# Hidden rows of an expert layer turned by way of DRAM and VectorE, with the second layer two slots behind

## The reference, cut to what matters

```python
e_idx = np.argmax(x @ w_gate, axis=1)              # x: 1536 x 512
for e in range(8):
    mask = e_idx == e
    h = np.maximum(x[mask] @ w1[e], 0.0)           # w1[e]: 512 x 1024
    ye = h @ w2[e]                                 # w2[e]: 1024 x 512
    out[mask] = gate_w[mask, None] * eom[mask, e, None] * ye
```

## Time and profile before

| | |
|---|---|
| median of 3 runs | 767.78 us (767.4 to 767.9) |
| span of the profiled execution | 765.7 us |
| TensorE busy | 754.3 us, 99% |
| VectorE, ScalarE, GpSimd busy | 421.5, 345.6, 368.7 us |
| expert stage (TensorE, first `layer1` to last `layer2`) | about 253 to 494 us |

### The profile page before, as it was taken

How to read it: one execution, slowest core, us unless ns; L and a number is a source line. 1 busy time by engine, 2 the same in 40 slices (tenths; PEclk the granted TensorE clock), 3 DMA queues, 4 the chain that set the end, 5 groups by cost and what they waited for, 6 DMA issues and landing times.

```text
span 765.7 us, 12544 instructions
## 1 busy us (share of the span) xinstructions
PE 754.3 (99%) x4243; PEld 630.2 (82%) x4243; DVE 421.5 (55%) x842; ACT 345.6 (45%) x658; POOL 368.7 (48%) x253
## 2 busy tenths in 40 slices
PE   8999999999999999999999999999999999999996
PEld 7677777777776788888888888998899889989985
DVE  8777777777765645444444545588147126414710
ACT  7766677777764313442244210285047117404610
POOL 5866567878721899777887860244200120010001
PEclk9999999999999999999999999999999999999998
DMA  4534333222111867755675611520200010000000
GB/s 112 128 97 121 92 81 100 57 59 57 28 45 27 324 205 255 219 182 184 213 246 157 233 54 32 194 92 1 61 22 1 29 56 1 0 28 15 1 14 28
DMA packets 42781, 73.70 MB, mean 96 GB/s; under 512 B 20352, under 2 KB 24096, under 8 KB 42720
## 3 DMA queue, kind: packets, MB, share of 16 engines
q1 hardware_dynamic: 29632, 30.05, 13.4%
q10 hardware_dynamic: 9584, 31.53, 12.4%
q0 software_dynamic: 3504, 11.30, 4.6%
HBM read 60.48 MB, written 11.28 MB: 94 GB/s over the span
## 4 chain that ended last, share of the span: by engine, by line
PE 62%; issue 29%; POOL 2%; DVE 2%; ACT 2%; DMA 1%; SPq 0%; POOLq 0%; DVEq 0%
PE pair_s L1478 14%; PE pair_t L1493 14%; PE pair_u L1284 8%; PE bank_b L1299 8%; PE pair_s L1271 5%; PE pair_t L1271 4%; PE pair_u L1453 2%; PE bank_b L1324 1%; POOL out L646 1%; PE pair_s L1531 1%; DVE g_lo L1213 1%; PE bank_a L1240 1%; POOL y_raw L640 1%; POOL w_part L518 1%; PE bank_a L1444 1%
## 5 line engine op out<-in xcount | busy, mean ns | idle before, releaser
L518 POOL TENSOR_TENSOR w_part<-w_raw,w_part 128x1024 fp32r<-128x1024 f32 x80 | 190.2, 2408 | 57.5 <-ACT w_part L756 57.3
L756 ACT ACTIVATE w_part<-w_raw 128x1024 fp32r<-128x1024 f32 x72 | 73.9, 1054 | 126.4 <-PE pair_t L1493 101.4
L1580 PE MATMUL pair_t<-w_part,g_hi 128*128 128x512 f32 x384 | 119.0, 391 | 0.3 <-POOL w_part L518 0.3
L646 POOL DMA_INDIRECT out<-o_sb,token x12 | 11.8, 985 | 208.5 <-DVE o_sb L1183 208.5
L1493 PE MATMUL pair_t<-w_part,hid_t 128*128 x456 | 109.0, 394 | 0.0
L1478 PE MATMUL pair_s<-w_part,xs_t 128*128 x456 | 108.7, 394 | 0.2 <-issue 0.2
L1478 PEld LDWEIGHTS pair_s<-w_part,xs_t 128*128 128x128 f32 x456 | 84.3, 188 | 17.7 <-issue 0.9
L1493 PEld LDWEIGHTS pair_t<-w_part,hid_t 128*128 128x128 f32 x456 | 84.4, 189 | 16.8
L859 ACT ACTIVATE elu<-elu 128x384 f32<-128x384 f32 x64 | 33.6, 525 | 122.9 <-DVE elu L1203 122.8
L698 ACT ACTIVATE exps<-exps,nmax 128x768 f32<-128x768 f32 x96 | 88.5, 925 | 0.6 <-DVE exps L916 0.6
L1580 PEld LDWEIGHTS pair_t<-w_part,g_hi 128*128 128x128 f32 x384 | 71.6, 188 | 15.1 <-issue 0.7
(11 more groups left out here) (219 smaller groups left out, 1088.3 us busy)
## 6 DMA issues: line engine op xcount, KB each, us to landing
w_raw<-in_moe_w ACTq DMA_DIRECT2D x48, 512.0 KB, 6.2
w_raw<-in_moe_w SPq DMA_DIRECT2D x16, 512.0 KB, 5.6
ys_sorted<-ys SPq DMA_DIRECT2D x19, 256.5 KB, 3.6
w_raw<-in_moe_w_in ACTq DMA_DIRECT2D x8, 512.0 KB, 5.7
raw<-in_q SPq DMA_DIRECT2D x16, 192.0 KB, 3.1
raw<-in_k SPq DMA_DIRECT2D x16, 192.0 KB, 3.3
v_nat<-in_v SPq DMA_DIRECT2D x16, 192.0 KB, 2.6
x_rows<-rows_sb SPq DMA_DIRECT2D x32, 96.0 KB, 2.3
```

The lines of the kernel that those rows point to most:

```text
L518: pool.tensor_tensor(chunk_of(w_part, n, 1, c), w_raw[n % 2][c][:, :], chunk_of(w_part, n, 0, c).bitcast(F32), ALU.subtract).then_inc(s_wl ...
L756: act.activation(chunk_of(w_part, n, 0, c), w_raw[n % 2][c][:, :], ACT.Copy).then_inc(s_whi, 1)
L1580: mm = pe.matmul(pair_t[:, t % 2, :], gp[:, f, j * P:(j + 1) * P], w_out_p[:, wp, f, :], start=f == 0 and m == 0, stop=f == FT - 1 and m == 2)
```

## The change

The eight transposes of the hidden rows leave TensorE. Instead SP stores `hid` to DRAM in four DMAs of 32 rows each (128 KB), waits until they have landed, and reads it back in one DMA of 512 KB into `hid_q`, arranged so that each group of 32 partitions holds one quarter of the hidden columns, for all rows. VectorE then transposes 32x32 blocks in place, copies the high part and subtracts the low part, all from and to SBUF. `hid_t` gets a second copy, `xs_raw` becomes a ring of 11 slots, and `layer2` lags two slots instead of one. ScalarE rounds chunks 0 to 3 of expert n ahead of its wait for layer 2 of expert n-2; on GpSimd the later gathers stand between chunks 3 and 4.

```diff
-AHEAD = {2: (), 3: (14,), 4: (15,), 5: (16,), 6: (17,), 7: (18,)}
+AHEAD = {2: (12, 13, 14), 3: (15,), 4: (16,), 5: (17,), 6: (18,), 7: ()}
+RING = 11
+LAG = 2
+QUAD = 32
+SOON_SLOTS = RING - NEXT_SLOTS
...
+        h_dram = nc.dram_tensor("h_quads", [2, P // QUAD, QUAD, P // QUAD, F1 // 4], F32).ap()
...
-            xs_raw = sb("xs_raw", [P, SLOTS, DM])
+            xs_raw = sb("xs_raw", [P, RING, DM])
-            hid_t = sb("hid_t", [P, 2, CF * P], F32R)
+            hid_q = sb("hid_q", [P, F1])
+            hid_t = sb("hid_t", [P, 2, 2, CF * P], F32R)
...
-            for n in range(SLOTS):
+            def hidden_quads(s):
+
+                sp.wait_ge(s_h, s + 1)
+                for g in range(P // QUAD):
+                    sp.dma_start(h_dram[s % 2, :, :, g, :].rearrange("q c f -> c q f"),
+                                 hid[g * QUAD:(g + 1) * QUAD, :].rearrange("c (q f) -> c q f", q=P // QUAD)).then_inc(s_hst, 16)
+                sp.wait_ge(s_hst, 16 * (P // QUAD) * (s + 1))
+                if s >= 1:
+                    sp.wait_ge(s_hte, 2 * s)
+                sp.dma_start(hid_q[:, :], h_dram[s % 2].rearrange("q c g f -> (q c) (g f)")).then_inc(s_hq, 16)
+
+            for s in range(SLOTS + LAG):
+                if s < SLOTS:
+                    hidden_quads(s)
+                n = s - LAG
+                if n < 0:
+                    continue
...
             for c in range(NCH):
                 w_lo(1, c)
-                gather_x(NEXT_SLOTS + c)
+                if c < SOON_SLOTS:
+                    gather_x(NEXT_SLOTS + c)
+            gather_x(RING)
             for n in range(2, E):
-                for s in AHEAD[n]:
-                    gather_x(s)
                 for c in range(NCH):
+                    if c == NC1:
+                        for s in AHEAD[n]:
+                            gather_x(s)
                     w_lo(n, c)
...
-                        if c in (0, NC1):
-                            wait_release(act, n, c, ends)
                         if c == NC1:
                             for i in range(NC1):
                                 w_hi(n, i)
+                        if c in (0, NC1):
+                            wait_release(act, n, c, ends)
...
             def relu(s):
                 if s >= 1:
-                    dve.wait_ge(s_ht, 2 * s)
+                    dve.wait_ge(s_hst, 16 * (P // QUAD) * s)
...
+            def turn_h(s):
+
+                if s >= 2:
+                    dve.wait_ge(s_l2, s)
+                dve.wait_ge(s_hq, 16 * (s + 1))
+                dve.transpose(hid_q[:, :].rearrange("p (g a e) -> p g e a", e=CF, a=QUAD),
+                              hid_q[:, :].rearrange("p (g a e) -> p g e a", e=CF, a=QUAD)).then_inc(s_ht, 1)
+                turned = hid_q[:, :].rearrange("p (g c e) -> p e g c", e=CF, c=QUAD)
+                dve.wait_ge(s_ht, s + 1)
+                dve.tensor_copy(hid_t[:, s % 2, 0, :].rearrange("p (e g c) -> p e g c", e=CF, c=QUAD), turned).then_inc(s_hte, 1)
+                dve.wait_ge(s_hte, 2 * s + 1)
+                dve.tensor_tensor(hid_t[:, s % 2, 1, :].rearrange("p (e g c) -> p e g c", e=CF, c=QUAD), turned,
+                                  hid_t[:, s % 2, 0, :].bitcast(F32).rearrange("p (e g c) -> p e g c", e=CF, c=QUAD),
+                                  ALU.subtract).then_inc(s_hte, 1)
...
-                copy_ht(s)
                 if s >= 1:
-                    copy_y(s - 1)
+                    turn_h(s - 1)
+                if s >= LAG:
+                    copy_y(s - LAG)
+            for t in range(BT):
+                take_yt(t)
+            turn_h(SLOTS - 1)
+            copy_y(SLOTS - LAG)
...
-            for s in range(SLOTS + 1):
+            for s in range(SLOTS + LAG):
...
-                if s >= 1:
-                    layer2(s - 1, of[s - 1][0], of[s - 1][2], 2 if s == SLOTS - 1 else None)
-                if s < SLOTS:
-                    turn_h(s)
+                if s >= LAG:
+                    layer2(s - LAG, of[s - LAG][0], of[s - LAG][2], 2 if s == SLOTS else None)
```

More of the change, by code:

```diff
@@ L348, in program @@
         s_h = sem("s_h")
+        s_hst = sem("s_hst")
+        s_hq = sem("s_hq")
         s_ht, s_hte = sem("s_ht"), sem("s_hte")
@@ L1103, in relu @@
                                   ALU.max).then_inc(s_h, 1)
-            def copy_ht(s):
-                if s >= 1:
-                    dve.wait_ge(s_l2, s + 1)
-                for half in range(2):
-                    to = slice(half * 512, (half + 1) * 512)
-                    dve.wait_ge(s_ht, 2 * s + half + 1)
-                    dve.tensor_copy(hid_t[:, 0, to], ring[2 + half]).then_inc(s_hte, 1)
-                    dve.wait_ge(s_hte, 4 * s + 2 * half + 1)
-                    dve.tensor_tensor(hid_t[:, 1, to], ring[2 + half], hid_t[:, 0, to].bitcast(F32),
-                                      ALU.subtract).then_inc(s_hte, 1)
+            def turn_h(s):
[11 more added lines that the diff above has]
+                                  ALU.subtract).then_inc(s_hte, 1)
             def copy_y(s):
@@ L1443, in turn_x @@
                     to = ring[c // 2] if s == 0 else ring[s % 2]
-                    mm = pe.transpose(to[:, c * P:(c + 1) * P], xs_raw[:, s, c::CD], ident)
+                    mm = pe.transpose(to[:, c * P:(c + 1) * P], xs_raw[:, s % RING, c::CD], ident)
                 mm.then_inc(s_xt, 1)
-            def turn_h(s):
-                pe.wait_ge(s_h, s + 1)
-                for half in range(2):
-                    if s >= 1:
-                        pe.wait_ge(s_hte, 4 * (s - 1) + 2 * half + 2)
-                    for c in range(4):
-                        mm = pe.transpose(ring[2 + half][:, c * P:(c + 1) * P], hid[:, half * 4 + c::CF], ident)
-                    mm.then_inc(s_ht, 1)
             def expert(s):
@@ L1492, in layer2 @@
                         a = CD * F1 + c * DM
-                        mm = pe.matmul(pair_t[:, s % 2, :], hid_t[:, hp, c * P:(c + 1) * P],
+                        if c == 0 and hp == 1:
+                            pe.wait_ge(s_hte, 2 * s + 2)
+                        mm = pe.matmul(pair_t[:, s % 2, :], hid_t[:, s % 2, hp, c * P:(c + 1) * P],
                                        w_part[:, bass.ds(par, 1), wp, a:a + DM],
```

20 lines of the change are left out of this document (9 added, 11 removed).

## The result

The changed kernel takes **804.67 us** (median of 4 runs, 799.5 to 806.1) against 767.64 for the kernel before (767.4 to 767.9, taken beside it): ratio 1.0469, 95% interval 1.0438 to 1.0501. It is slower, as forecast, but by 37 us where 9 were forecast, and outside the range of 764.5 to 791.

What follows compares the result with a forecast made beforehand. TensorE, busy 99% of the span, was taken to bound the kernel. 765.7 - 15.4 (transposes) + 5.0 (fill) + 19.8 (late weights) = 775.1 span, plus 2.1 to the median: 777.2 us, range 764.5 to 791.

Steps and rivals of the forecast that it cites:

- What goes: TensorE, expert stage: 19 times eight transposes of hidden rows leave, saving 15.4 us; the beat becomes 11.52 us.
- Filling: Pipeline start, slots 1 and 2: TensorE waits for x, expert 1's weights and the first hidden store, costing 5.0 us.
- Weights: Layer 1 of experts 3, 5 and 7: the second lag makes weights 6.6 us late each, 19.8 us in all.
- Port: SBUF port: VectorE's copy and subtraction hold up GpSimd's subtractions by 2.0 us a slot, 4.0 per expert.
- Hidden otherwise: VectorE, store and read-back: 6.5 to 11.3 us of VectorE work per slot and the trip fit, costing nothing.
- Clock: TensorE at the three weight waits: clock falls, half a block lost per wait, 785.5 us; chance 0.25.
- the main case: Whole kernel: transposes saved, less fill and three late weight waits, gives 777.2 us, 1.2% slower; chance 0.45.
- VectorE becomes the bound: VectorE per slot: 32-byte steps cost double, making 12.1 us a slot, 0.6 over the beat; 788 us; chance 0.10.
- Port free: SBUF port: VectorE slips into GpSimd's gaps at no cost, three waits of 2.6 us, 765.2 us; chance 0.12.
- never late: Expert weights: early rounding keeps ahead, so layer 1 does not wait for them, 757.4 us; chance 0.05.

Runs made afterwards that it cites:

- e6_keep_busy: The changed kernel with 16 identity matmuls added on TensorE ahead of layer 1 of slots 6, 10 and 14; 797.79 us, ratio 1.0371 to the kernel before.
- e2_order: The changed kernel with first-layer chunks of expert n+1 loaded, rounded and subtracted before second-layer chunks of expert n; 820.04 us, ratio 1.0682 to the kernel before.
- e4_stt: The changed kernel with VectorE's copy of the turned rows written as a scalar_tensor_tensor of the same values; 816.15 us, ratio 1.0636 to the kernel before.
- e1_psum: The changed kernel with the block transpose writing a free PSUM pair, which copy and subtraction then read; 782.02 us, ratio 1.0194 to the kernel before.
- e12_sbuf2: The changed kernel with the transpose writing a second SBUF buffer that copy and subtraction read in runs without gaps; 791.41 us, ratio 1.0337 to the kernel before.

## Why the prediction was wrong

**What goes**: right. 152 matmul instructions fewer, beat 11.39 us (11.52 forecast).

**Filling, 5.0 us**: its waits were 4.9 (1.05 and 3.85), by the way through the store on SP that I had bounded at 4.7; the slow blocks behind them add 3.2, and the first layer 2 waits 3.6 more for turned rows, which no term held. Part of the 3.2 varies between executions: in e6_keep_busy the block of slot 1 is not slow behind the same wait.

**Weights, 19.8 us**: the mechanism, the three places (slots 6, 10, 14) and the path hold. 29.4 us from release to layer 1, 29.6 forecast: 6.9 to the first subtraction (5.5 forecast), 22.3 for the eight (18.9 + 4.0 for the port forecast), no gather between. That the sums agree within 0.2 is partly luck: the first part was 1.4 short, and I had counted 1.2 for a gather among the eight, where the code puts it ahead of them. The lateness is 4.9 and not 6.6 because the two beats had themselves grown to 24.5, by turned rows that were late (1.28 and more at 323.42). Measured 14.6. Before slot 10 GpSimd stands 1.71 us for a rounded chunk between the fourth and the fifth subtraction, so the loads are part of that path already.

**Port, 4.0 an expert**: that the two exclude each other held, and the 3.1 us by which GpSimd's eight were stretched before slot 6 is near. What failed is the other direction. I let VectorE wait for one GpSimd instruction, "up to 2.4 of waiting for GpSimd at each of the two". That is so in most slots, but in three of the nineteen the copy waits to the end of the run, up to 9.74 us, and in e2_order a subtraction stands 20.34; these few make TensorE's longest waits for rows. The Trainium skill ("SBUF — State Buffer", section "Who interferes with whom") says that the shared ports are an exclusive lock, held for the whole instruction. The traces agree for single instructions (2.80 us in the earlier trace rows, 3.25 at 409.06 in e4_stt); 9.74 and 20.34 us are more than one. What it says of VectorE with at most one SBUF input, outside its two-port modes, agrees with 1.22 us throughout in e1_psum.

**Hidden otherwise, 0 us**: this is the step that failed. "The store and read-back, some 5 + 6 us, with 0.7 of copy, fit in the 23 us between relu and layer 2" took the copy at its work, and left the waiting that a sentence before it bounded at 2.4 us out of the way to layer 2. It also let the read-back follow the store at once, where it waits for the single `hid_q`: 150.8 us of SP's waits, and a loop of 12.5 us or more when the read-back takes 7. The transpose takes 2.2 us (estimate 1.2, bound 2.4), the copy 1.1 at best (0.7), the subtraction 2.0 (1.3): 2.1 us more a slot before any waiting, and the waiting comes on top. It cost 14.2 us of waits and part of the slow blocks; e1_psum gives 22.7 us back, the port's share of the weights' path included. How the 14.2 divide between the port and the single `hid_q` no run separates.

**Rivals.** *Clock* (0.25): it happened, beside the main case and not in place of it. I priced one half block for each of three waits, 8.3 us; ten blocks lost 18.6, since there were many more waits. The rule of the Trainium skill ("TensorE: Matmul & The Clock Gate", section "What's actually happening") that idleness lowers the clock and activity restores it agrees with e6_keep_busy, 5.72 us where the changed kernel has 7.67. *VectorE becomes the bound* (0.10): its premise, the 32-byte steps, was true (1.10 against 0.69 us, 2.02 against 1.22 in e12_sbuf2) and its 788 was the nearest of the cases, but VectorE still waits for TensorE and the transfers 59 us of the stage; what bounds is the moment of its copy, not its load. The Trainium skill, "SBUF — State Buffer", section "Door 1", on 16-byte lines agrees for these two. For the transpose only the writing was varied (2.22 us in place, 2.14 into whole runs); it reads in steps of 32 bytes in every run, so whether its reads pay is not shown. *Port free* and *never late*: excluded by the 14.6 us.

The cases were priced as alternatives. They came together, and by the timelines one lateness fed the next: behind the late weights of slots 6 and 10 GpSimd's next eight subtractions stood against VectorE's copy, the late copy made TensorE stand again, and standing cost clock.

Left open: how the 18.6 us of slow blocks would split if each wait were removed alone, what decides whether VectorE is let in between two subtractions, what a second `hid_q` with the trip would give, why the single store is slower, and whether a lag of three would hide the trip. Neither the second `hid_q` nor the lag of three was run.

## What to carry to other kernels

Work moved off a full engine pays only as far as the next path allows: compute each other path's length per beat (here release to weights, 28 to 29 us, against two beats) before counting the saving. Do the same for each loop that a single buffer closes (here read-back, transpose, copy, subtraction). An operation that shares a resource with another engine can wait for the whole uninterrupted run on the other side, so bound it by that run and not by one instruction; reading from PSUM avoided it here. A wait put on a full TensorE costs its length and often a slow block behind it: 4.87 us cost 2.1 more, 1.28 us at 323.42 nothing.

## What was not expected of the hardware

- A VectorE copy or subtraction with SBUF inputs can stand to the end of a back-to-back run of GpSimd's: 9.74 us beside a run of 18.84, 20.34 beside one of 18.45, and GpSimd is not slowed meanwhile. In other slots it is let in after one instruction and GpSimd pays: 3.25 us at 409.06 in e4_stt, beside a run of eight that took 23.74. A 32x32 transpose from SBUF to SBUF does not stand: 2.25 us at 343.82, inside the same run.
- Either form can wait so, `tensor_copy` 9.74, `scalar_tensor_tensor` 10.05.
- SBUF reads in steps of 32 bytes: copy 1.10 us against 0.69 in whole runs, subtraction 2.02 against 1.22 (128x1024). From PSUM in whole runs each takes 1.22.
- The block transpose of 128x1024 in fp32, reading in steps of 32 bytes, takes 2.0 to 2.3 us wherever it writes; a relu of that size from PSUM takes 1.22.
- Sixteen SBUF-to-SBUF transfers cost 10.0 to 11.6 us of one queue to issue.
